# A scan stage whose partitions hold four consecutive tokens instead of one token of each of four tiles

## What is computed

```python
f = lower_bound + (1 - lower_bound) * sigmoid(f_logit)
for t in range(S):                       # S = 5056, for each of 2 batches
    h = f[:, t] * h + (1 - f[:, t]) * x[:, t];  y[:, t] = h
x = y.reshape(10112, 256)
# layer 1: logits = unit(x) @ unit(expert_emb).T / tau;  layer 2: logits = x @ w_gate
e = argmax(logits); gate = softmax(logits)[e]
out = gate * (relu(x @ w1[e]) @ w2[e])   # each token through its own expert only
```

## Time and profile before

| | us |
|---|---|
| median of 3 runs (lowest, highest) | 1435.62 (1434.92, 1435.73) |
| the profiled execution, whole | 1434.47 |
| its span in the trace | 1432.7 |
| scan stage, first transposition to last logits, in the trace | 8 to 121 |
| routing of layer 1 in the trace | 121 to 171 |

### The profile page before, as it was taken

How to read it: one execution, slowest core, us unless ns; L and a number is a source line. 1 busy time by engine, 2 the same in 40 slices (tenths; PEclk the granted TensorE clock), 3 DMA queues, 4 the chain that set the end, 5 groups by cost and what they waited for, 6 DMA issues and landing times.

```text
span 1432.7 us, 32311 instructions
## 1 busy us (share of the span) xinstructions
PE 1341.3 (94%) x10937; PEld 1298.1 (91%) x10937; DVE 973.9 (68%) x1373; ACT 837.3 (58%) x1393; POOL 472.2 (33%) x481
## 2 busy tenths in 40 slices
PE   6994799999999999999999388999999999999996
PEld 6893399999999999999999238999999999999996
DVE  5788566666666666666666765777777777777773
ACT  4673266666666666666666125666666666666663
POOL 3465531122122112211220263444444444444441
PEclk9796599999999999999999658999999999999998
DMA  8991675656565566556663067666666666666650
GB/s 266 290 318 56 71 256 186 212 194 205 195 212 191 196 203 208 199 192 203 203 205 114 8 22 260 219 220 215 220 222 219 222 225 217 227 224 220 223 184 1
DMA packets 204616, 276.42 MB, mean 193 GB/s; under 512 B 33334, under 2 KB 171972, under 8 KB 204580
## 3 DMA queue, kind: packets, MB, share of 16 engines
q1 hardware_dynamic: 191044, 240.74, 54.2%
q0 software_dynamic: 13536, 35.21, 7.3%
HBM read 242.69 MB, written 35.18 MB: 194 GB/s over the span
## 4 chain that ended last, share of the span: by engine, by line
PE 84%; issue 7%; DVE 3%; POOL 2%; DMA 2%; ACT 1%; SPq 0%; ACTq 0%; POOLq 0%; DVEq 0%
PE bank L1105 37%; PE bank L1123 36%; PE bank L1089 3%; PE bank L1077 2%; PE bank L1134 2%; PE bank L1143 1%; POOL vals L766 1%; PE bank L1041 1%; PE bank L1028 1%; PE bank L1047 1%; DMA w2raw<-in_moe_w 1%; ACT sq L907 1%; DVE hT L344 1%; DVE gx L334 1%; DMA xb<-rows_b,row_i 0%
## 5 line engine op out<-in xcount | busy, mean ns | idle before, releaser
L1105 PE MATMUL bank<-xs,w1h 128*128 128x256 f32 x3008 | 570.0, 288 | 3.0 <-DVE xs L511 3.0
L950 ACT ACTIVATE hh<-bank 128x512 fp32r<-128x512 f32 x376 | 225.3, 599 | 417.9 <-PE bank L1105 417.9
L1105 PEld LDWEIGHTS bank<-xs,w1h 128*128 128x128 f32 x3008 | 461.9, 190 | 3.8 <-DVE xs L511 3.8
L522 DVE SCALAR_TENSOR_TENSOR hl<-bank,hh 128x512 fp32r<-128x512 f32 x376 | 260.1, 692 | 265.2 <-ACT hh L950 262.5
L1123 PE MATMUL bank<-w2h,hl 128*128 128x256 f32 x1504 | 423.8, 282 | 0.0
L1105 PE MATMUL bank<-xs,w1l 128*128 128x256 f32 x1504 | 423.3, 281 | 0.0
L1123 PE MATMUL bank<-w2l,hh 128*128 128x256 f32 x1504 | 423.0, 281 | 0.0
L1123 PE MATMUL bank<-w2h,hh 128*128 128x256 f32 x1504 | 422.5, 281 | 0.0
L1105 PEld LDWEIGHTS bank<-xs,w1l 128*128 128x128 f32 x1504 | 285.3, 190 | 0.0
L1123 PEld LDWEIGHTS bank<-w2h,hh 128*128 128x128 f32 x1504 | 283.9, 189 | 0.0
L1123 PEld LDWEIGHTS bank<-w2l,hh 128*128 128x128 f32 x1504 | 283.7, 189 | 0.0
(11 more groups left out here) (117 smaller groups left out, 1068.3 us busy)
## 6 DMA issues: line engine op xcount, KB each, us to landing
w1raw<-in_moe_w SPq DMA_DIRECT2D x94, 1024.0 KB
w2raw<-in_moe_w SPq DMA_DIRECT2D x94, 1024.0 KB, 5.5
rows_b<-yb SPq DMA_DIRECT2D x94, 128.0 KB, 1.8
xin<-in_x SPq DMA_DIRECT2D x19, 512.0 KB, 6.4
fin<-in_f_logit SPq DMA_DIRECT2D x19, 512.0 KB, 8.6
rows_a<-h_rows SPq DMA_DIRECT2D x19, 512.0 KB, 6.1
xb<-rows_a,row_i POOLq DMA_INDIRECT x94, 4.5
xb<-rows_b,row_i POOLq DMA_INDIRECT x94, 5.2
```

The source lines that it names most:

```text
L522: v.scalar_tensor_tensor(hl[:, j, :], bank[j][:, :], 0.0, hh[:, j, :].bitcast(fp32), ALU.max, ALU.subtract).then_inc(hid_lo, 1)
L950: nc.scalar.activation(hh[:, j, :], bank[j][:, :], ACT.Relu).then_inc(hid_hi, 1)
L1105: ins = mm(bank[j][:, f * GW:(f + 1) * GW], w[:, p, o:o + P], xs[:, p, a, c * GW:(c + 1) * GW], start=k == 0, stop=k == 3 * DC - 1)
```

## The change

A partition of a chunk now holds four consecutive tokens, `512*k + 4*p + j` for j = 0..3. A load has 128 runs of 4 KB. The transposes of the front are as before and leave token `4*q + j` of the chunk in column `128*j + q` of its bank. The order of time is restored when the banks are read: the tanh and `gx` read their bank with the innermost step of 128 columns (four elements, 512 bytes apart, then the next), and write contiguously. The scan, `fg` and `hT` stay in the order of time. The transposes back and the logits take as weights every fourth column of `hT` (a step of 16 bytes), so that partition and `j` of the rows agree with the load. The last chunk has three tokens to a partition. The token number by partition and tile is made by two iotas in place of one; the three instructions that computed `slot_tok` go away, and `pair` takes the token numbers from `meta`, which came with the gathered rows.

```diff
-    x_v = x.rearrange("b s d -> (b s) d").rearrange("(t p) d -> p t d", p=P)
-    f_v = f_logit.rearrange("b s d -> (b s) d").rearrange("(t p) d -> p t d", p=P)
+    x_t = x.rearrange("b s d -> (b s) d")
+    f_t = f_logit.rearrange("b s d -> (b s) d")
+    NW = TT // CH
+    def chunk_of(t, k, nt):
+        if nt == CH:
+            return t[0:NW * CW, :].rearrange("(k p j) d -> k p j d", p=P, j=CH)[bass.ds(k.value(), 1), :, :, :
+                                                                              ].rearrange("o p j d -> p (o j d)")
+        return t[NW * CW:N, :].rearrange("(p j) d -> p (j d)", j=nt)
+    def in_time(ap2, nt):
+        return ap2.rearrange("p (j q) -> p q j", j=nt)
+    def by_token(ap2, nt):
+        return ap2.rearrange("p (q j) -> p q j", j=nt)
...
-                    v.scalar_tensor_tensor(gx[:, c, 0:w], fg[:, c, 0:w], 1.0, bank[c][:, 0:w],
+                    v.scalar_tensor_tensor(by_token(gx[:, c, 0:w], nt), by_token(fg[:, c, 0:w], nt), 1.0,
+                                           in_time(bank[c][:, 0:w], nt),
...
-                        link(v.tensor_copy(pair[:, 0:T, 1], tok_a[:, :] if m == 0 else slot_tok[:, :]))
+                        link(v.tensor_copy(pair[:, 0:T, 1], tok_a[:, :] if m == 0 else
+                                       meta[:, :].rearrange("p (t w) -> p t w", w=2)[:, :, 1]))
...
-                    link(v.scalar_tensor_tensor(small[:, TMP_R, :], v0, float(P), v1,
-                                                ALU.mult, ALU.add))
...
-                    link(v.scalar_tensor_tensor(small[:, OUT_R, :], empty[:, :], float(N + 1),
-                                                small[:, TMP_R, :], ALU.mult, ALU.add))
-                    link(v.tensor_scalar(slot_tok[:, :], small[:, OUT_R, :], -1.0, None, ALU.add))
...
-                k0 = k.value(CH)
-                for dst, src in ((xin, x_v), (fin, f_v)):
-                    sp.dma_start(dst[:, slot_x, 0:nt * D].rearrange("p (t d) -> p t d", d=D),
-                                 src[:, bass.ds(k0, nt), :]).then_inc(xf_in[slot_x], 16)
+                for dst, src in ((xin, x_t), (fin, f_t)):
+                    sp.dma_start(dst[:, slot_x, 0:nt * D], chunk_of(src, k, nt)).then_inc(xf_in[slot_x], 16)
...
-            const(pool.iota(tok_a[:, :], pattern=[[P, TT]], base=0, channel_multiplier=1,
+            const(pool.iota(tok_a[:, 0:NW * CH], pattern=[[CW, NW], [1, CH]], base=0, channel_multiplier=CH,
                             allow_small_or_imprecise_dtypes=True))
+            const(pool.iota(tok_a[:, NW * CH:TT], pattern=[[1, TT - NW * CH]], base=NW * CW,
+                            channel_multiplier=TT - NW * CH, allow_small_or_imprecise_dtypes=True))
...
-                    nc.scalar.activation(th[:, c, 0:w], bank[2 + c][:, 0:w], ACT.Tanh,
+                    nc.scalar.activation(by_token(th[:, c, 0:w], nt), in_time(bank[2 + c][:, 0:w], nt), ACT.Tanh,
...
-                                                  hT[:, c, par, j * P:(j + 1) * P], ident[:, :])
+                                                  by_token(hT[:, c, par, 0:nt * P], nt)[:, :, j], ident[:, :])
...
-                        ins = mm(bank[6][:, j * E:(j + 1) * E], hT[:, c, par, j * P:(j + 1) * P],
+                        ins = mm(bank[6][:, j * E:(j + 1) * E], by_token(hT[:, c, par, 0:nt * P], nt)[:, :, j],
```

More of the change, by code:

```diff
@@ L129, in build @@
         slot_row = sb("slot_row", [P, ST], i32)
-        slot_tok = sb("slot_tok", [P, ST], fp32)
         empty = sb("empty", [P, ST], fp32)
@@ L270, in build @@
         CHUNKS_A, CHUNKS_B = -(-TT // RC), -(-ST // RC)
-        POOL_CONST = 13
+        POOL_CONST = 14
         LOOP_K = 6
@@ L495, in routing @@
                 mark["experts", m] = count[0]
-                if m == 0:
-                    link(v.scalar_tensor_tensor(small[:, OUT_R, :], empty[:, :], float(N + 1),
-                                                small[:, TMP_R, :], ALU.mult, ALU.add))
-                    link(v.tensor_scalar(slot_tok[:, :], small[:, OUT_R, :], -1.0, None, ALU.add))
             def run_ap(t, b, T):
```

## The result

| | before | changed |
|---|---|---|
| median of the runs | 1435.67 us (4 runs, 1434.92 to 1437.21) | 1491.07 us (4 runs, 1488.82 to 1493.47) |
| ratio | | 1.0395, 95% interval 1.038 to 1.041 |
| profiled execution (span) | 1434.47 (1432.7) | 1488.82 (1487.0) |

The account below looks back on a forecast made before the run. The scan was taken as balanced between TensorE's work and the ScalarE/VectorE chain. 1434.5 - 1.0 (loads) + 8.6 (bank reads) - 0.1 (small things) = 1442.0, so 1443 for the runs' median; range 1431 to 1480, the forecast's own 1438 to 1455.

Parts of the forecast that it names:

- What bounds the kernel: Scan stage: balanced between TensorE's own work, 4.62 us a turn, and the chain through ScalarE and VectorE, 4.70; measured 4.82.
- Part 3: Back transposes and logits: weights from every fourth column of `hT`, 24 loads a chunk, taken to cost 0.
- The other end: Upper bound for strided weight loads, at the moving side's price: 234 ns a load, +2.9 us a chunk.
- its two cases: TensorE's clock under costly weight loads: full, a turn of 7.5 us; lower (0.50), some 8.6 us, time up to 1495.
- Part 2: Scan: gx and tanh read banks with a 512-byte step, +0.32 us each, +8.6 us in sum.
- The row of the reduction: Profile row of a VectorE reduction over 632 spread inputs, 1211 against 811 ns; source of the bank reads' price.
- Rival A: Scan's bank reads are as fast with a step as without: 1434.5 us, between 1431.5 and 1436.5; chance 0.28.
- Part 1: Loads in 4 KB runs: -0.6 us at the start, -0.4 us of ScalarE's wait for the first expert's weights.
- the cover: In the scan's steady part nothing waits for a load, so faster loads are worth 0 there.
- Part 4: Small things: routing instruction removed, -0.25 us at most; second iota at the start, +0.15; changed token slots, 0.
- B: Scan's strided weight loads pay the moving side's price: turn 7.5 us, time 1477, up to 1495 at lower clock; chance 0.31.
- rival C: First expert's weights come earlier, ending ScalarE's 5.0 us of waits and the slow-clock stretch: -8 us, 1427.6; chance 0.06.

## Why the prediction was wrong, by its steps

**What bounds the kernel.** Right, and it is why the error was so large: the scan was balanced, TensorE's own work at 4.62 us in a turn of 4.82, so a price on TensorE had no slack to fall in.

**Part 3, the step that failed.** "By the row of the same operation I take 0." The row compared recorded durations of weight loads at half clock, 146 and 151 ns, beside matmuls of 344 ns. It measured how long the record of a load is when something else sets the pace. The prediction named both weak points, and then gave the row its value all the same. Half clock hid much too: at the lower level an fp32 load with 16 bytes between columns shows 20 ns of its 121 (233 against 213). The other end that it had worked out, "128 x 1.83 = 234 ns a load", from the moving side of the same matmuls, is what the chip takes: 233 ns from one piece to the next, in the kernel and alone. Of the 24 strided operands in a chunk only the 16 pieces of logits pay, 3.63 - 1.70 = +1.9 us; the eight transposes pay 11 ns each, which the other end had wrong.

The 46 us of the scan add up from the starts in the trace. Put down each stretch from one matmul's start to the next to the line of the first, with idle time apart. From the first front to the last logits the stage is 112.5 us before and 158.8 in the changed kernel:

| us | before | changed | |
|---|---|---|---|
| logits | 37.1 | 71.0 | +33.9 |
| fronts | 44.2 | 59.0 | +14.7 |
| transposes back | 21.0 | 26.4 | +5.4 |
| TensorE idle | 10.2 | 2.4 | -7.8 |

So the strided loads themselves are +34 us. The fronts and the transposes back add 20, and that is the lower clock but for the 11 ns of the transposes: 204 of the 316 front pieces ran at the lower level, at 213 ns from one to the next for 109, where 40 did before. Idle time takes in 8. The remark "If TensorE, now mostly waiting within its loads, were granted the lower clock" came true at 0.72 to 0.74, between its two cases; "a turn would be some 8.6 us" stands against 8.05. With the 8 us of the addresses the sum is 1435.7 + 46 + 8 = 1490, against 1491.07.

The Trainium skill (SBUF — State Buffer, "Door 1: The DMA port swizzle") was weighed in that part with both its halves. The first half, full rate from two accesses to a line of 16 bytes, agrees with the loads of fp32 weights at the full clock: two columns in 16 bytes take 118 ns against 112, and steps of 12 and 16 bytes 174 and 233 ns. The second half, four fp32 as a free stride, is contradicted by 233 ns against 112. For the transposes neither holds as a price: 120 against 109 ns.

**Part 2.** Wrong, +8.6 predicted and next to nothing found. `gx` is at 687 and the tanh at 598 ns, where 1000 and 920 were named. The row of the reduction is of a read in SBUF with another instruction, and it does not carry over to a bank. Rival A had this mechanism right. In sum: with all weights in a row the changed kernel is at 1443.15 (ratio 1.0063), and the kernel before with an unused tile of 128 bytes, which moves the same tiles by as much modulo 256, at 1442.49 (1.0059). The loads, the bank reads and the smaller routing together are worth 0.7 us, within the spread of these runs.

**Part 1.** Right in the cover, and nearly nothing in size: -1.0 predicted, nothing measurable found. That the loads come faster is not shown: ScalarE waits 3.0 and 1.3 us for the first expert's weights with the logits in a row, 2.8 and 2.1 with both in a row, where it was 3.2 and 1.8.

**Part 4.** "Tokens change slots: 0 (bounds -1 to +1)" holds for the slots. The step that was missing is the removed tile: that it moves `xb`, `xs`, `hh`, `hl` and all behind them. I counted the instructions that `slot_tok` took with it and not its 384 bytes. This alone is +8 us, of the 14 by which the time is above B's 1477. The rest is what the lower clock costs (some 20 us, the table above) less what B had counted for the transposes, which don't pay.

**The rivals.** B is what happened, with 16 of its 24 operands paying, and the lower clock and the addresses on top. It had 0.31 and the forecast 0.33; the range to 1480 covered its plain form and not the one with the lower clock, which the text itself gave 1495. Of rival C, earlier weights alone give -4.3 us of the -8 it was priced at, and that the slow stretch came from these waits is not shown. In the changed kernel its waits are gone too, where TensorE covers all.

## What to carry to other kernels

A strided matmul operand is cheap or dear by what it hides behind: take its price from pieces that follow each other with little to hide it, as last start less first start by the count, with the clock level of the stretch beside it, and not from the recorded duration of a load next to a wide matmul. When a bound from a nearby row of the same engine is larger by tens of microseconds and the stage has no slack, it deserves more than the value at nothing. For fp32 weights keep two neighbouring columns in each 16 bytes, or put the stride on the side that reads the bank, which cost next to nothing here; and when a tile is removed or added, look at where the operands behind it now begin.

## What the runs showed of the hardware that was not expected

- The fp32 weights of a matmul with 16 bytes between columns take 233 ns a load at either level of the clock; in a row they take 112 at the full clock and 213 at the lower. With 8 and 12 bytes they take 118 and 174 at the full clock and 213 at the lower. fp32r weights take 235 against 119 even under 256 moving columns.
- Transposes whose input has the same step take 120 against 109 ns, and that shows in no kernel's time. The price does not grow with the step (120, 113, 120, 112 at 8, 12, 16 and 32 bytes). Why they differ from a matmul, and whether their strided operand is loaded as weights at all, as the prediction took it, the runs don't tell.
- ScalarE and VectorE read a bank of PSUM with 512 bytes from element to element within 2% of a contiguous read (598 and 687 ns for 512 elements, 597 and 675 in a row).
- TensorE with no idle time in the record was granted 0.73 with 8 moving columns and 1.00 with 256, in series of 7.3 and 7.5 us with loads of the same length.
- Tiles moved by 128 bytes modulo 256 cost up to 8 us, 0.6% of the kernel (+5 us for 96, nothing for 256). 6 of the 8 lie in the matmuls whose weights are `hh` and `hl`, also where `xb` and `xs` stay in place. The mechanism is open.
